# Block attention and two matrix stages on one core: a turning transfer asked for earlier, a copy placed later, a smaller memset

## The reference, cut to what matters

```python
batch, n_heads, seq, head_dim = (2, 8, 768, 64); block, window = (32, 16)
k_sum = k.reshape(B, H, nb, block, D).max(axis=3)            # nb = 24 blocks
v_sum = v.reshape(B, H, nb, block, D).mean(axis=3)
scores_l = scale * q @ k.T, kept where |i - j| < window
scores_s = scale * q @ k_sum.T + log(block)
a = softmax(concatenate([scores_l, scores_s]))
y = a @ concatenate([v, v_sum])                              # all tokens: 1536 x 512
h = np.maximum(y @ w_in, 0.0); x = h * h @ w_out             # 512 -> 2048 -> 512
# second stage 512 -> 1024 -> 512: h * softmax(h), layer norm, w_out
```

## Time and profile before

| | us |
|---|---|
| median of 3 runs | 462.12 (461.55 to 462.47) |
| the profiled execution, its own time | 462.32 |
| its span | 460.5 |
| TensorE busy | 452.2 |
| VectorE busy | 261.1 |
| ScalarE busy | 210.8 |
| GpSimd busy | 77.7 |
| granted TensorE clock | 1.0 of full speed throughout |

### The profile page before, as it was taken

How to read it: one execution, slowest core, us unless ns; L and a number is a source line. 1 busy time by engine, 2 the same in 40 slices (tenths; PEclk the granted TensorE clock), 3 DMA queues, 4 the chain that set the end, 5 groups by cost and what they waited for, 6 DMA issues and landing times.

```text
span 460.5 us, 6612 instructions
## 1 busy us (share of the span) xinstructions
PE 452.2 (98%) x2470; PEld 371.2 (81%) x2470; DVE 261.1 (57%) x441; ACT 210.8 (46%) x473; POOL 77.7 (17%) x67
## 2 busy tenths in 40 slices
PE   8989999999999999999999999999999999999997
PEld 6778877888888888888888888888888888888885
DVE  2997868886645434434224233344657676767630
ACT  2897646756733544444323333333342435343521
POOL 2420021110100000000000000000125335533520
PEclk9999999999999999999999999999999999999999
DMA  8997689584412722200131111211143433353341
GB/s 281 302 271 228 212 216 314 174 202 107 81 24 71 209 63 63 65 6 19 24 92 47 46 48 54 61 67 46 46 93 58 80 69 68 81 119 77 68 114 46
DMA packets 67903, 49.64 MB, mean 108 GB/s; under 512 B 48160, under 2 KB 52896, under 8 KB 67872
## 3 DMA queue, kind: packets, MB, share of 16 engines
q1 hardware_dynamic: 67872, 49.23, 39.5%
HBM read 33.82 MB, written 5.24 MB: 85 GB/s over the span
## 4 chain that ended last, share of the span: by engine, by line
PE 89%; DVE 4%; ACT 2%; DMA 2%; issue 2%; POOL 0%; SPq 0%; DVEq 0%; ACTq 0%; POOLq 0%
PE bank L1040 26%; PE bank L1068 26%; PE bank L1184 14%; PE bank L1166 14%; PE bank L960 3%; PE bank L1017 2%; DMA probsT_in<-halves 2%; ACT probs L536 1%; PE bank L966 1%; PE bank L985 1%; DVE probs L743 1%; DMA k_raw<-kT 1%; DVE k_sum L718 1%; PE bank L1077 1%; DVE probs L761 1%
## 5 line engine op out<-in xcount | busy, mean ns | idle before, releaser
L774 DVE TENSOR_TENSOR sqr<-relu 128x512 f32<-128x512 f32 x48 | 33.1, 690 | 91.9 <-ACT relu L601 91.9
L601 ACT ACTIVATE relu<-bank 128x512 f32<-128x512 f32 x48 | 28.7, 597 | 114.1 <-PE bank L1040 113.2
L1040 PE MATMUL bank<-x_hi,win_hi 128*128 128x512 f32 x192 | 76.4, 398 | 0.0
L1068 PE MATMUL bank<-h_hi,wout_hi 128*128 128x512 f32 x192 | 75.1, 391 | 0.0
L1040 PE MATMUL bank<-x_hi,win_lo 128*128 128x512 f32 x192 | 74.9, 390 | 0.0
L1040 PE MATMUL bank<-x_lo,win_hi 128*128 128x512 f32 x192 | 74.9, 390 | 0.0
L1068 PE MATMUL bank<-h_hi,wout_lo 128*128 128x512 f32 x192 | 74.7, 389 | 0.0
L1068 PE MATMUL bank<-h_lo,wout_hi 128*128 128x512 f32 x192 | 74.7, 389 | 0.0
L520 POOL COPY planes<-cen 128x2048 uint16<-128x2048 uint16 x12 | 33.6, 2799 | 169.5 <-PE bank L1068 113.8
L536 ACT ACTIVATE probs<-probs,neg_max 128x120 f32<-128x120 f32 x96 | 36.6, 382 | 23.2 <-DVE neg_max L747 23.1
L1040 PEld LDWEIGHTS bank<-x_hi,win_lo 128*128 128x128 f32 x192 | 36.0, 188 | 7.6
(11 more groups left out here) (82 smaller groups left out, 714.1 us busy)
## 6 DMA issues: line engine op xcount, KB each, us to landing
win_raw<-w_in_t SPq DMA_DIRECT2D x8, 512.0 KB, 6.0
q_sb<-qT SPq DMA_DIRECT2D x16, 256.0 KB, 4.0
wout_raw<-w_out_t SPq DMA_DIRECT2D x8, 512.0 KB, 6.6
win_raw<-w_t SPq DMA_DIRECT2D x8, 512.0 KB, 3.6
v_ext<-vwin SPq DMA_DIRECT2D x16, 192.0 KB, 4.2
out<-o_sb SPq DMA_DIRECT2D x12, 256.0 KB, 2.9
k_ext<-kT SPq DMA_DIRECT2D x12, 192.0 KB, 4.0
k_raw<-kT SPq DMA_DIRECT2D x4, 400.0 KB, 5.9
```

The costliest lines, as they stand in the source:

```text
L601: nc.scalar.activation(relu[:, :], up_bank(n), ACT.Relu).then_inc(relu_ok, 1)
L774: nc.vector.tensor_tensor(sqr[:, n % 3, :], relu[:, :], relu[:, :], ALU.mult)\
L1040: last = nc.tensor.matmul(up_bank(n), win[a][:, f * WC + k * P:f * WC + (k + 1) * P], x[b][:, c % 2, k * CH:(k + 1) * CH], start=(k == 0 a ...
L1068: last = nc.tensor.matmul(down_bank(d), wout[a][:, f * WC + d * P:f * WC + (d + 1) * P], h[b][:, n % 3, :], start=(f == 0 and a == 0 and b ...
```

## The change

SP asks for the turning of unit u + 2 right behind the queries and key windows, ahead of load_vn, of the raw weights and of the spreading of v_sum. POOL's copy of the block means waits in addition for `norm_ok` to reach 8, the norm of unit 7. The memset of `halves` clears only the last 8 of 128 columns of each of its 8 slices, which the split never writes.

```diff
@@ block.sync, loop over u
                 if UPB <= u + PPB + 2 < UNITS:
                     load_kw(u + PPB + 2)
+                if u + 2 < UNITS:
+                    turn_probs(u + 2)
                 if u < UPC + VP - 1:
                     load_vn(u - UPC + 1)
                 if u < UPB:
...
                     sp.dma_start(g_sb[:, :], g_cols).then_inc(g_in, 16)
-                if u + 2 < UNITS:
-                    turn_probs(u + 2)
@@ block.gpsimd
-            nc.gpsimd.memset(halves[:, :, :, :], 0)
+            nc.gpsimd.memset(halves[:, :, :, KX:], 0)
             windows_k(0)
...
             windows_k(UPC + 1)
+
+            pool.wait_ge(norm_ok, UPC)
             pool.wait_ge(vmean_ok, PPB)
             nc.gpsimd.tensor_copy(v_ext[0:NB, :, :], ...).then_inc(vkept_ok, 1)
```

## The result

| | before | changed kernel |
|---|---|---|
| median, us | 461.74 (460.65 to 462.47, 6 runs) | 465.48 (465.11 to 467.28, 6 runs) |
| span of the profiled execution | 460.5 | 464.8 |
| its own time | 462.32 | 466.6 |
| mean granted TensorE clock | 1.0 | 0.993 |

The ratio is 1.0096 with a 95% interval of 1.008 to 1.0111: slower by 4.4 us on 461.7 by the ratio, 3.7 us by the medians. The forecast was +2.3 us (464.4 us), in a range from 462.3 to 466.4.

What follows compares the result with a forecast made beforehand. TensorE, busy 98% of the span, was taken to bound the kernel. Copy -0.78, late v_next +1.52 (turning's 1.40 gain already spent) and further VectorE delays +1.54 gave +2.28 us: 464.4 us, range 462.3 to 466.4.

Steps and rivals of the forecast that it cites:

- The copy: POOL's copy moved behind unit 7's norm: VectorE's norm of unit 5 takes 0.66 us, not 1.44; -0.78 us.
- The memset: On POOL before its key copies: a shorter memset only lengthens the wait for keys; 0 us.
- The gain of the earlier turning: TensorE's waits of 0.40, 0.20 and 0.80 us around units 10 and 11 go: 1.40 us to be had.
- load_vn(2) would cost VectorE 1.3 us: This v_next load, now behind unit 11's turning, comes at 71.5, not 70.3: VectorE loses 1.3 us, TensorE nothing yet.
- The wait for load_vn(3): VectorE waits a whole round of 5.7 us behind norm(12); up(8) starts at 85.85, +1.52 us with 1.40 spent.
- The knock-on: VectorE late before values(12), scores(14) and up(9): +0.57, +0.40, +0.57, in all +1.54 us; estimated 0 to 1.6.
- a gap of about 3 us ahead of up(8): Sign of being right: TensorE waits there, released by win_lo; below 1 us would show the forecast wrong.
- A: Rival: load_vn(3) is hidden and only removed waits count; -2.2 us, 459.9 us; chance 9%.
- B: Rival: a draw, VectorE reaches norm(12) at 77.0 and unseen slack takes the later waits; -0.3 us, 461.8; chance 15%.
- C: Rival: copy's 0.78 us swallowed in ScalarE's wait, v_next needs 4.8 to 5.4 us; +4.6 us, 466.7; chance 14%.
- The lock: VectorE with two SBUF inputs and GpSimd lock the shared port pair exclusively; norm(5) takes 1.44 us for 0.66.
- The estimate for the 384 KB of v_next: About 2 us plus bytes over 436 GB/s: 2.9 us to land; with it the sum would be 0.4 us less.

Runs made afterwards that it cites:

- experiment 2: Kernel before, with only POOL's copy of the means also waiting for the norm of unit 7: 460.71 us, ratio 0.9981.
- experiment 3: Kernel before, with only the memset of halves made smaller: 461.47 us, ratio 0.9999.
- experiment 4: Kernel before, with SP asking for load_vn, then the turning, then the weights; POOL as before: 461.02 us, ratio 0.9987.
- experiment 5: Kernel before, with the turning ahead of load_vn, weights and spreading in loop turn u = 10 alone: 467.06 us, ratio 1.0117.
- experiment 6: Changed kernel, with load_vn(3) alone put back ahead of the turning of unit 12: 459.55 us, ratio 0.9957.
- experiment 9: Changed kernel, with the two weights of loop turn u = 10 asked for behind the spreading: 465.97 us, ratio 1.0108.
- experiment 7: Changed kernel, with 17 more products on TensorE between down(5) and up(8), into a bank nobody reads: 464.49 us, ratio 1.0063.
- experiment 8: Changed kernel, with load_vn first, then the turning; weights of u = 9 wait for u = 10, between load_vn(3) and the turning: 458.92 us, ratio 0.9937.
- experiment 1: Kernel before, with the change's order of transfers alone, POOL's copy and memset as before: 466.44 us, ratio 1.0106.

## Why the prediction was right, and where its sizes were off

**The copy** was right in mechanism and size: norm(5) at 0.65 us, -0.78 forecast, -0.72 in the trace and -0.8 by the medians of experiment 2, whose own trace keeps less of it.

**The memset** was right: 0 (experiment 3).

**The gain of the earlier turning** was right in place. 1.40 us were put down; 1.26 came in the changed kernel, where 0.21 us are left ahead of values(11), and 1.55 in experiment 4, whose load_vn(2) stands ahead of the turning (VectorE waited 1.0 us for it). The forecast said that load_vn(2) would cost VectorE 1.3 us and TensorE nothing; it cost 1.72 and 0.21.

**The wait for load_vn(3)** was the step that decided, as forecast, and experiments 5 and 6 show it. Its size was low: 5.7 us forecast, 6.76 measured. Split, hand-overs and issue came out as summed (76.54 + 0.66 to 79.56 is 2.36 us, forecast 2.38). The landing did not: 4.37 us where 3.3 was taken. That 3.3 was the landing of load_vn(1) in the trace of before, the shortest of four: idle DMA engines, no turning ahead of it, and the weights right behind. With a turning ahead load_vn(3) took 3.9 to 4.4 us in the five kernels that have it so. What the turning adds can be read from load_vn(1), for which the engines are idle in every trace but for the turning: 3.2 to 3.6 us in the seven kernels that ask for it before the turning, 4.0 us in the five that ask for it behind, and 0.25 us of this is SP's own issue (0.57 to 0.58 us for 0.33). The weights behind it are no full rival, since load_vn(1) had them behind it in the trace of before and landed in 3.3; with them taken away load_vn(3) still took 3.9 (experiment 9). The trace of before had no row with a turning ahead, and between its ends of 3.3 and 5.4 the shorter was chosen.

From values(11) to up(8) there are 4.33 us more than before, against 1.52 + 1.40 = 2.92 forecast. Not all of this is the landing. Laid on the time of before by values(9) (1.32 us), norm(12) ended at 78.5 and not at 78.0, and up(8) started at 87.4 and not at 85.85: 1.55 us late, of which 1.1 is the landing and 0.5 the later norm(12), held back by load_vn(2), whose wait had been put at 1.3.

**The knock-on** of 1.54 us was right where the clock holds: 1.55 us in experiment 7, at the three places named (values(12), scores(14), up(9)), and `win_lo` of tile 9 held by POOL's split, 1.50 us where 1.22 was given. In the changed kernel itself it does not show.

**The clock** was missing from the sum. The prediction read a gap of about 3 us ahead of up(8) and priced it at its own length. In its place the runs showed a gap of 4.15 us behind which TensorE worked at half speed, 2.56 us, of which 1.0 is net of the knock-on (0.2 in the traces of experiments 5 and 9). The trace of before has a clock of 1.0 throughout and no gap over 1.3 us between TensorE's instructions, so no row could price it; but a gap three times the longest one seen should have carried an upper bound.

By the terms: -0.78 - 1.40 + 2.92 + 1.54 = +2.28 forecast; -0.72 - 1.26 + 4.33 + 2.56 = +4.91 in this pair of traces, less the 0.60 of the head. The profiled execution is one of the slower ones; on the medians the change is +3.7. Of the rivals, A and B are out: the load was not hidden and no slack took the knock-on. C (466.7 us) named a landing of 4.8 to 5.4 us and the copy's gain swallowed, and said that it decides from a landing over 4 us. The landing came to 4.4, past that point; the copy's gain was not swallowed.

That 465.48 us lies in the range is in part luck. It is 1.1 us above the 464.4 that was summed, about halfway to C, and by the ratio (+4.4 us) it is nearer to C than to the sum. The upper end of the range was set by a longer landing. The slow clock had no part in it and came on top, and the range was wide enough for both.

What the prediction cited holds with one note. The lock that it took from the Trainium skill, SBUF — State Buffer, on the engine ports agrees with all runs: 1.40 to 1.44 us for norm(5) in the four profiled kernels of the experiments that keep the early copy, 0.65 in the six that move it and in the changed kernel. The estimate for the 384 KB of v_next by the Trainium skill, SBUF — State Buffer, on how bandwidth depends on size, 2.9 us, was met by none; the fastest landing was 3.2 us, on idle engines. The Trainium skill, TensorE: Matmul & The Clock Gate, in its part on HAM oscillation, describes a wait for DMA after which the engine starts at the low clock; the changed kernel and experiment 7 agree, with up(8) at 5.4 us behind the gap and 2.9 (85.60 to 88.46) when it is filled. In experiment 5 up(8) still began at the full clock.

## What to carry to other kernels

Before a transfer that waits is moved ahead in an in-order queue, list what it now stands in front of, and for each of these ask whether its consumer is a condition of the wait: here the load of v_next was needed by the instruction right behind the one that the turning waits for, which turned a prefetch into a round trip from VectorE through GpSimd, SyncE and the DMA engines. The same load can be lost a second way, by bytes ahead of it on full DMA engines; the order that won (experiment 8) asks for the small load with a near deadline ahead of both the waiting transfer and the large loads with far deadlines. Price a new gap of TensorE of some microseconds above its length, and a landing by a row with the same neighbours ahead of it, not by the shortest.

## What the runs showed of the hardware

- After a gap of 4.15 us TensorE's granted clock was at the 1.2 GHz level for the next 5 us of work (12 products in 5.40 us, before 2.72); after 1.3 us, the longest gap in the trace of before, it had stayed at 2.4 GHz. The gap of 4.04 us in experiment 5 had the fall later, after the gap (0.93 in 86 to 88 us, 0.50 in 88 to 90). From up(8) to up(9) it took 9.62 and 9.71 us in two traces (changed kernel, experiment 1) and 8.81 and 8.82 in two others (5, 9), with the clock held up 8.61 (experiment 7).
- A load of 384 KB landed in 3.2 to 3.6 us on idle engines, in 3.9 to 4.4 us with a turning DMA asked for 1.3 us ahead of it (load_vn(1) in 4.0, load_vn(3) in 3.9 to 4.4), and in 8.0 to 8.3 us behind 1 MB of weights.
- The first 28 us vary by up to 1.75 us between executions of the same instructions, 1.4 us of it in six idle products that took 2.93 us in one trace and 1.56 in eleven. The shift is carried to values(9): from values(3) it is 30.28 to 30.30 us in all five traces that keep the early copy. Effects under 1 us need the distance between two points in TensorE's line, not the span.
